# Dynamic convolution and gated MLP: head of the kernel reordered, and copies of weight rows issued later

## What is computed

```python
w = softmax(weight_gen, axis=-1)
conv[b, s, h, :] = sum(w[b, s, h, k] * x_pad[b, s + k, h, :] for k in range(7))
h = conv.reshape(16384, 192) @ w_in          # 192 x 2048
g = h * sigmoid(1.702 * h)
out = g @ w_out                              # 2048 x 192
```

## Time and profile before

| | before |
|---|---|
| median of 3 runs | 1126.83 us (1126.73 to 1127.22) |
| profiled execution, its own time | 1126.67 us |
| span of its trace | 1124.9 us |
| TensorE busy | 1111.5 us (99%) |
| VectorE / ScalarE / GpSimd busy | 802.1 / 622.0 / 12.8 us |
| bytes moved | 43.46 MB, mean 39 GB/s |

### The profile page before, as it was taken

The page is one execution under the profiler, slowest core; times in us unless marked ns, Lnnn a source line. Parts: engine busy times, 40 slices in busy tenths (PEclk is TensorE's granted clock), DMA queues, the critical chain, the costliest instruction groups (busy, mean ns, idle before and its releaser), DMA issues.

```text
span 1124.9 us, 21696 instructions
## 1 busy us (share of the span) xinstructions
PE 1111.5 (99%) x9748; PEld 915.3 (81%) x9748; DVE 802.1 (71%) x710; ACT 622.0 (55%) x661; POOL 12.8 (1%) x13
## 2 busy tenths in 40 slices
PE   6999999999999999999999999999999999999998
PEld 4888888888888888888888888888888888888886
DVE  7999988687685966859668496785858768587322
ACT  7767655464645555455464554645555555454543
POOL 2100000000000000000000000000000000000000
PEclk9999999999999999999999999999999999999999
DMA  8801010101001010010100101010010100100000
GB/s 274 238 15 54 15 54 1 39 29 40 29 2 39 29 40 29 1 57 12 40 29 18 51 1 40 29 40 29 1 40 29 40 29 1 40 29 1 29 1 29
DMA packets 9980, 43.46 MB, mean 39 GB/s; under 512 B 1120, under 2 KB 2400, under 8 KB 7584
## 3 DMA queue, kind: packets, MB, share of 16 engines
q1 hardware_dynamic: 8400, 40.51, 10.9%
q0 software_dynamic: 1488, 1.57, 0.9%
HBM read 24.77 MB, written 12.58 MB: 33 GB/s over the span
## 4 chain that ended last, share of the span: by engine, by line
PE 98%; DVE 1%; DMA 0%; issue 0%; ACTq 0%; DVEq 0%; SPq 0%; ACT 0%
PE hid L655 47%; PE acc_main L671 31%; PE acc_rest L671 21%; DMA gate<-in_x_first 0%; DVE hid L489 0%; DVE prod L483 0%; PE acc_main L622 0%; DVE hid L483 0%; DVE outs_main L511 0%; ACTq L73 0%; DVE outs_rest L552 0%; DVEq L73 0%; PE acc_rest L622 0%; SPq L199 0%; ACT outs_main L304 0%
## 5 line engine op out<-in xcount | busy, mean ns | idle before, releaser
L317 ACT ACTIVATE gate<-hid 128x1024 f32<-128x1024 f32 x256 | 263.1, 1028 | 480.0 <-PE hid L655 479.4
L568 DVE TENSOR_TENSOR gate_lo<-gate,gate_hi 128x1024 fp32r<-128x1024 f32 x256 | 312.9, 1222 | 260.6 <-ACT gate_hi L320 260.5
L655 PE MATMUL hid<-xt,w_hi 64*128 64x512 f32 x3072 | 431.5, 386 | 0.0
L655 PEld LDWEIGHTS hid<-xt,w_hi 64*128 64x128 f32 x3072 | 287.7, 184 | 61.6 <-ACT gate_hi L320 0.8
L671 PE MATMUL acc_main<-gate_hi,w 64*128 64x512 f32 x2048 | 315.8, 386 | 0.0
L320 ACT ACTIVATE gate_hi<-hid 128x1024 fp32r<-128x1024 f32 x256 | 260.7, 1018 | 0.0
L671 PEld LDWEIGHTS acc_main<-gate_hi,w 64*128 64x128 f32 x2048 | 191.9, 184 | 40.3
L655 PE MATMUL hid<-xt,w_lo 64*128 64x512 f32 x1536 | 215.8, 386 | 0.0
L671 PE MATMUL acc_rest<-gate_hi,w 64*128 64x512 f32 x1024 | 199.6, 386 | 0.0
L671 PE MATMUL acc_rest<-gate_lo,w 64*128 64x512 f32 x1024 | 199.6, 386 | 0.0
L671 PE MATMUL acc_main<-gate_lo,w 64*128 64x512 f32 x1024 | 199.6, 386 | 0.0
(11 more groups left out here) (57 smaller groups left out, 229.7 us busy)
## 6 DMA issues: line engine op xcount, KB each, us to landing
xwin<-in_x_runs SPq DMA_DIRECT2D x15, 1056.0 KB, 4.9
out<-outs_main SPq DMA_DIRECT2D x13, 512.0 KB, 2.6
out<-outs_rest SPq DMA_DIRECT2D x13, 256.0 KB, 2.9
taps<-in_tap_runs SPq DMA_DIRECT2D x1, 3136.0 KB, 10.4
taps<-in_w_rows SPq DMA_DIRECT2D x2, 1536.0 KB, 9.6
w_hi<-w_hi SPq DMA_DIRECT2D x2, 768.0 KB, 10.4
w_lo<-w_lo SPq DMA_DIRECT2D x2, 768.0 KB, 8.7
out<-outs_main SPq DMA_DIRECT2D x6, 256.0 KB, 2.0
```

The lines of the kernel that those rows point to most:

```text
L317: nc.scalar.activation(gate[:, v % 2, :, :], hid[:, v % 2, :, :], ACT.Gelu_apprx_sigmoid).then_inc(gate_ready, 1)
L568: nc.vector.tensor_tensor(gate_lo[:, v % SLOTS, :, :], gate[:, v % 2, :, :], gate_hi[:, v % SLOTS, :, :], ALU.subtract).then_inc(gate_lo_r ...
L655: last = nc.tensor.matmul(hid[:, v % 2, h, :], w[rows, k if j else slice_of(h, k), q, f], xt[rows, j % 2, part, k, :], start=(i == 0), sto ...
```

## The change

TensorE takes over part of the head's sum. It multiplies VectorE's product 0 (its first 512 columns) and GpSimd's three products by the identity and accumulates them in PSUM (`head_pile`); GpSimd's addition goes, and its third product is made in two halves. VectorE adds its products 1 and 2, then product 0's last 256 columns, then product 3, and the closing sums add this to the pile. The identity is loaded with `x_first`, as 128 more columns. The warm-up is 16 matmuls of 128 columns of zeros, which GpSimd sets first. All three rounded slices of piece 0 are written by ScalarE; unit 0 takes its terms slice by slice; its `gate_hi` is a copy of its gate, and unit 2 waits for the gate alone. `w1` is rounded in two halves, and GpSimd, not ScalarE, negates the later half, in two parts with a transfer each. The early remainder of `w2` moves from unit 2 to unit 1 on VectorE. On SP, the `w1_hi` copies move behind the wait for the late remainders, in front of the `w1_lo` copies.

```diff
-WARM_UP = 4
+WARM_UP = 16
...
-        head_prod = [prod[:, k, 0:N_FIRST] for k in range(2)]
-        shared_prod = [prod[:, 0, N_FIRST:N_CONV], prod[:, 1, N_FIRST:N_CONV], conv[:, 0:N_FIRST]]
+        first_flat = gate[:].rearrange("p b h n -> p (b h n)")[:, 0:FIRST_WIN * D + P]
+        ident = first_flat[:, FIRST_WIN * D:FIRST_WIN * D + P]
+        head_prod = [prod[:, 0, 0:N_FIRST], prod[:, 0, N_FIRST:N_CONV], prod[:, 1, 0:N_FIRST]]
+        head_sum = prod[:, 1, N_FIRST:N_CONV]
+        shared_prod = [conv[:, 0:N_FIRST], conv[:, N_FIRST:N_CONV], head_more[:]]
...
-            sp.dma_start(x_head, x_first).then_inc(x_loaded, 16)
+            sp.dma_start(first_flat, x_first).then_inc(x_loaded, 16)
...
-            sp.dma_start(ident[:], identity).then_inc(ident_loaded, 16)
...
-            sp.wait_ge(w1_hi_ready, 1)
+            sp.wait_ge(w1_lo_ready, 3)
+            sp.wait_ge(w1_late_ready, 2)
+            sp.wait_ge(w1_hi_ready, 2)
             sp.dma_start(w1_hi[LOWER, :, 1, :].bitcast(F32), w1_hi[UPPER, :, 0, :].bitcast(F32)).then_inc(w1_doubled, 16)
             sp.dma_start(w1_hi[UPPER, :, 1, :].bitcast(F32), w1_hi[LOWER, :, 0, :].bitcast(F32)).then_inc(w1_doubled, 16)
-            sp.wait_ge(w1_lo_ready, 3)
-            sp.wait_ge(w1_late_ready, 2)
...
-            nc.scalar.activation(w1_hi[:, :, 0, :], w1_raw, ACT.Copy).then_inc(w1_hi_ready, 1)
-
-            act.wait_ge(w1_hi_ready, 1)
-            nc.scalar.activation(w1_lo[:, :, 0, LATE], w1_hi[:, :, 0, LATE].bitcast(F32), ACT.Copy, scale=-1.0
-                                 ).then_inc(w1_negated, 1)
+            for cols in (EARLY, LATE):
+                nc.scalar.activation(w1_hi[:, :, 0, cols], w1_raw[:, :, cols], ACT.Copy).then_inc(w1_hi_ready, 1)
...
-            for k in (0, 2):
+            for k in range(SLICES):
                 act.wait_ge(head_turned_ready, k + 1)
-                nc.scalar.activation(xt[:, 0, 0, k, :], head_turned[k], ACT.Copy).then_inc(head_hi_act, 1)
+                nc.scalar.activation(xt[:, 0, 0, k, :], head_turned[k], ACT.Copy).then_inc(head_hi, 1)
...
+                    if n == 0:
+                        act.wait_ge(gate_ready, 1)
+                        nc.scalar.activation(gate_hi[:, 0, :, :], gate[:, 0, :, :], ACT.Copy).then_inc(gate_hi_ready, 1)
...
+                mul(0, head_prod[0])
+                mul(1, head_acc)
                 mul(2, head_prod[1])
+                mul(3, head_prod[2])
+                dve.wait_ge(head_op, 7)
+                add(head_acc, head_acc, head_prod[1])
+                dve.wait_ge(head_op, 9)
+                add(head_acc[:, N:N_FIRST], head_acc[:, N:N_FIRST], head_prod[0][:, N:N_FIRST])
                 dve.wait_ge(head_op, 10)
+                add(head_sum, head_acc, head_prod[2])
                 dve.wait_ge(head_op, 11)
+                dve.wait_ge(head_piled, 1)
...
-            dve.wait_ge(head_turned_ready, 2)
-            nc.vector.tensor_copy(xt[:, 0, 0, 1, :], head_turned[1]).then_inc(head_hi_dve, 1)
...
-                    if n == 2:
+                    if n == 1:
                         w2_remainder(2, SOON)
...
+            for i, first, last in ((0, 0, FIRST), (1, 0, FIRST), (2, 0, FIRST // 2), (2, FIRST // 2, FIRST)):
...
-            nc.gpsimd.tensor_tensor(shared_prod[2], shared_prod[1], shared_prod[2], ALU.add).then_inc(shared_op, 1)
-            pool.wait_ge(w1_negated, 1)
-            pool.dma_start(w1_raw[:, :, LATE], w1_lo[:, :, 0, LATE].bitcast(F32), accum_op=ALU.add).then_inc(w1_added, 16)
+            pool.wait_ge(w1_hi_ready, 2)
+            for i, part in enumerate(LATE_PARTS):
+                nc.gpsimd.tensor_scalar(w1_lo[:, :, 0, part], w1_hi[:, :, 0, part].bitcast(F32), -1.0, None,
+                                        ALU.mult).then_inc(w1_negated, 1)
+                pool.wait_ge(w1_negated, i + 1)
+                pool.dma_start(w1_raw[:, :, part], w1_lo[:, :, 0, part].bitcast(F32), accum_op=ALU.add
+                               ).then_inc(w1_added[i], 16)
...
+                for _ in range(WARM_UP):
+                    nc.tensor.matmul(head_turned[0][:, 0:P], zeros, zeros, start=True, stop=True)
                 pe.wait_ge(x_loaded, 16)
...
                 pe.wait_ge(head_op, 5)
+                pile(head_prod[0], FORE, start=True)
+                pe.wait_ge(shared_op, 1)
+                pile(shared_prod[0], FORE)
+                pile(shared_prod[0], AFT, start=True)
+                pe.wait_ge(shared_op, 2)
+                pile(shared_prod[1], FORE)
+                pile(shared_prod[1], AFT)
+                pe.wait_ge(shared_op, 3)
+                pile(shared_prod[2], slice(0, WAY))
+                pe.wait_ge(shared_op, 4)
+                pile(shared_prod[2], slice(WAY, N), stop=True)
+                pile(shared_prod[2], AFT, stop=True).then_inc(head_piled, 1)
...
-                wait(pe, gate_hi_ready, n - 1)
+                if n == 2:
+                    pe.wait_ge(gate_ready, 1)
+                else:
+                    wait(pe, gate_hi_ready, n - 1)
...
+                if n == 0:
+                    terms = [(w, 0, k) for k in range(SLICES) for w in (w1_hi, w1_lo)] + terms[2 * SLICES:]
```

More of the change, by code:

```diff
@@ L33 @@
 CROSS_HI_AT, CROSS_LO_AT = (7, 7, 5), (7, 7, 5)
-WARM_UP = 4
+WARM_UP = 16
 SHARED = 3
 def ffn_of_dynamic_conv(nc: bass.Bass, x_runs: bass.AP, tap_runs: bass.AP, x_first: bass.AP, tap_first: bass.AP,
-                        identity: bass.AP, w1_rows: bass.AP, w2_rows: bass.AP, out: bass.AP):
+                        w1_rows: bass.AP, w2_rows: bass.AP, out: bass.AP):
     CB = x_runs.shape[2]
@@ L172, in slice_of @@
             return (k + h) % SLICES
+        EARLY, LATE = slice(0, FH // 2), slice(FH // 2, FH)
+        LATE_PARTS = (slice(FH // 2, FH * 3 // 4), slice(FH * 3 // 4, FH))
         SOON = CH // 4
         LATE_CHUNKS = ((SOON, SOON + 2), (SOON + 2, CH // 2))
[L176 removed]
         MAIN, MAIN_LO = slice(0, P), slice(2 * P, 3 * P)
@@ L583, in _ @@
         def _(pool):
+            nc.gpsimd.memset(zeros, 0.0).then_inc(zeros_ready, 1)
             pool.wait_ge(x_loaded, 16)
             pool.wait_ge(head_shared, 1)
-            g = FIRST * H
-            norm = tap_norm[:, 0:g * SHARED].rearrange("p (g k) -> p g k", k=SHARED)
-            for i in range(SHARED):
-                k = ALONE + i
-                nc.gpsimd.tensor_tensor(shared_prod[i].rearrange("p (g c) -> p g c", c=GRP),
-                                        x_head[:, k:k + FIRST, :].rearrange("p t (h c) -> p (t h) c", c=GRP),
-                                        norm[:, :, i:i + 1].broadcast_to([P, g, GRP]), ALU.mult).then_inc(shared_op, 1)
-            pool.wait_ge(shared_op, SHARED)
-            nc.gpsimd.tensor_tensor(shared_prod[2], shared_prod[1], shared_prod[2], ALU.add).then_inc(shared_op, 1)
-            pool.wait_ge(w1_negated, 1)
-            pool.dma_start(w1_raw[:, :, LATE], w1_lo[:, :, 0, LATE].bitcast(F32), accum_op=ALU.add).then_inc(w1_added, 16)
+            norm = tap_norm[:, 0:FIRST * H * SHARED].rearrange("p (g k) -> p g k", k=SHARED)
+            for i, first, last in ((0, 0, FIRST), (1, 0, FIRST), (2, 0, FIRST // 2), (2, FIRST // 2, FIRST)):
+                k, of = ALONE + i, slice(first * H, last * H)
+                nc.gpsimd.tensor_tensor(shared_prod[i].rearrange("p (g c) -> p g c", c=GRP)[:, of],
+                                        x_head[:, k + first:k + last, :].rearrange("p t (h c) -> p (t h) c", c=GRP),
+                                        norm[:, of, i:i + 1].broadcast_to([P, (last - first) * H, GRP]), ALU.mult
+                                        ).then_inc(shared_op, 1)
+            pool.wait_ge(w1_hi_ready, 2)
[5 more added lines that the diff above has]
+                               ).then_inc(w1_added[i], 16)
             for i, (at, to) in enumerate(LATE_CHUNKS):
@@ L606, in turn_head, with pile @@
             def turn_head():
-                flat = x_head.rearrange("p t d -> p (t d)")
+                pe.wait_ge(zeros_ready, 1)
+                for _ in range(WARM_UP):
+                    nc.tensor.matmul(head_turned[0][:, 0:P], zeros, zeros, start=True, stop=True)
                 pe.wait_ge(x_loaded, 16)
+                FORE, AFT, WAY = slice(0, N), slice(N, N_FIRST), N_FIRST // 2
+                def pile(part, cols, start=False, stop=False):
+                    return nc.tensor.matmul(head_pile[:, cols], ident, part[:, cols], start=start, stop=stop)
                 pe.wait_ge(head_op, 5)
-                for i in range(WARM_UP):
-                    nc.tensor.matmul(hid[:, 0, 0, :], flat[:, i * P:(i + 1) * P], flat[:, N:2 * N], start=True, stop=True)
-                pe.wait_ge(ident_loaded, 16)
+                pile(head_prod[0], FORE, start=True)
[10 more added lines that the diff above has]
+                pile(shared_prod[2], AFT, stop=True).then_inc(head_piled, 1)
                 for k in range(SLICES):
@@ L621, in turn_head @@
```

(9 more changed lines are left out.)

57 lines of the change are left out of this document (23 added, 34 removed).

## The result

| | before | after |
|---|---|---|
| median | 1126.80 us (6 runs) | 1131.02 us (6 runs, 1130.82 to 1131.46) |
| profiled execution, its own time | 1126.67 us | 1131.27 us |
| span | 1124.9 us | 1129.5 us |

The ratio is 1.0036, with a 95% interval of 1.0027 to 1.0046: slower by 4.2 us. The prediction was 1132.0.

A forecast was written before the change was run, and what follows sets the result against it. TensorE, busy 99% of the span, was taken to bound the kernel. The median 1126.83 plus 5.1 us for the late window, already containing the head's 1.15 gain, gave 1131.9, stated as 1132.0; range 1129.5 to 1134.5.

The forecast's parts named there:

- The row copies: In SP's queue, the moved w1_hi copies delay piece 2's window to 64.2, making second product 14 5.1 us late.
- VectorE's 22.07 us in one piece: VectorE works without idle from piece 2's first product to unit 14's remainder; TensorE has 0.55 us of room there.
- the term 7.4 us: Delay of piece 2's window by two more w1_hi copies ahead in SP's queue: 1.57 MB at 213 GB/s.
- The head: The start of the kernel up to unit 4: the rearranged sum gives 1.1 to 1.2 us, ScalarE early by 1.15.
- the closing sums' 1.16: In the head, the closing sums start at 12.3 instead of 13.46, 1.16 us gained.
- 64 KB can cost only their share: The first load, grown from 960 to 1024 KB, takes nothing to 0.31 us more; 0.16 was taken.
- The wait of 0.3 before unit 4: In the head, TensorE was to wait about 0.3 us before unit 4, with ScalarE what is late next.
- A: Rival at SP's queue: the copies do not hold up piece 2's window, only the head counts, 1125.6; chance 0.10.
- B: Rival at SP's queue: the copies run at the rate of loads, 4.2 us, giving 1128.7; chance 0.09.
- C: Rival at second product 10: TensorE's clock falls in the new wait, 1132.0 to 1134.2; chance 0.15 for over 0.5 us.
- the 2.2 us of later waits: After the 4.0 us wait at second product 10, TensorE's shorter waits at units 11 and 14.
- D: Rival in the head: zeros do not raise the clock, the head loses 1.0 instead of winning 1.16, 1134.2; chance 0.06.

The follow-up runs named there:

- e2: The kernel before, with only both w1_hi copies moved behind the wait for the late remainders, in front of the w1_lo copies; 1132.65 us, ratio 1.0049.
- e5: The kernel before, with only the second w1_hi copy moved behind the wait for the late remainders; 1128.73 us, ratio 1.0017.
- e8: e3 with the identity loaded by a transfer of its own behind the first x; 1125.13 us, ratio 0.9986.
- e7: e3 with GpSimd's negations held back until VectorE has made the three early remainders of w1; 1125.68 us, ratio 0.9989.
- e1: The changed kernel with the two w1_hi copies issued early again, as soon as w1 is rounded; 1125.82 us, ratio 0.9989.
- e4: The changed kernel with the window of piece 2 issued ahead of the taps, the copies left in place; 1125.58 us, ratio 0.9989.
- e6: e3 without the 16 multiplications of zeros; 1127.44 us, ratio 1.0006 to the kernel before.
- e3: The changed kernel with all four copies of w1 rows issued behind the window of piece 2; 1125.84 us, ratio 0.9991.
- e10: The changed kernel itself measured and profiled once more, with nothing changed; 1131.18 us, ratio 1.0039.
- e9: e8 with e7's wait added, so the identity is loaded apart and the negations are held back; 1125.42 us, ratio 0.9988.

## Why the prediction was right, point by point

**The row copies: right, and the cost a little too high.** The way from SP's queue over the window, VectorE's 22.07 us in one piece and the 0.55 us of room to second product 14 held in all its steps: from 63.84 to the weight load of second product 14 at 85.97 it was 22.13, the 22.07 and the hand-over. What was mis-sized is the term 7.4 us. The window landed 5.85 later than before although it was issued 0.75 earlier, which makes the copies 6.6 us, 238 GB/s; by the same reckoning they cost 6.9 in e2 (landing at 65.16, with a first x 0.26 later), and e5's single one 3.1. Why they ran faster than the 213 GB/s of 16:22 is not shown. That stretch also held the end of piece 1's window, until about 17.6, but 18:20, behind it, gave 215 as well; after the change the four stretches of 2 us in 42:50 gave 221 to 233.

**The head: right in the steps, too good in the size.** It was put at 1.15 us and ScalarE showed 0.75 in the profiled execution. Of the closing sums' 1.16, 0.51 came; 0.60 is the first x, which landed at 6.7 instead of 6.1. That 64 KB can cost only their share was the weak step; the profiles with and without them differ by 0.3 on average, and single executions by more. Part of this was made good by luck: the first activation came 4.67 after the sums, not 4.93, so 0.24 were gained on ScalarE behind the sums where the prediction had nothing (0.14 - 0.15). The pile itself took what it should (7.83 to the sums at 12.95, 5.1 against 5.0), and it, not VectorE, set the sums, as said. In e8, where the first x came early, the head gave 1.6 at unit 4, with the stall of unit 1 absent too. The wait of 0.3 before unit 4 that was forecast is not in the changed kernel, since TensorE came later than ScalarE there.

**A wait not foreseen.** The negations were costed on GpSimd and on whoever waits for them, with a bound of 1.82 us (they took 2.14 and 2.66), but not on VectorE, which works beside them. The first of the two remainders took 1.67 us instead of 0.55. In the changed kernel that costs TensorE 0.34, and some 0.3 of it reaches unit 4 (28.53, where ScalarE would have let it load at 28.22). The sum did not suffer, because the window's landing hangs on ScalarE: SP issued the first copy 0.76 early, like gate_hi. In the kernels without the late window it is worth 0.3 by the rows (e7, e8).

**The two errors offset in part.** Cheaper copies took 0.8 us off and the later ScalarE put 0.4 on: 4.7 in the profiled execution instead of 5.1, and 4.2 by medians. That they have opposite signs is luck.

**The rivals.** A fell with e1, e2 and e4: the window could not overtake. B fell with the rate. C happened, and cost nothing. The stretch 68.5:72 after the wait of 3.2 us (instead of the 4.0 forecast), with the columns of the earlier trace rows:

```profile
68.50:72.00 3.50, 3.40 (x16) 2.71 (x18) 3.43 (x7) 2.68 (x4) 0.00 (x0) 0.51 0.00 0
```

The granted clock was 0.51, the lower level, and second product 10 took 3.7 us until the next first product instead of 2.3; the extra 1.4 and the 0.76 that TensorE still waited at unit 14 are together the 2.2 us of later waits that the prediction had left to it. In e5, with waits of 1.1 and 1.2 us, the clock stayed at 1.00; in e2, after 3.75 us, it stood at 1.00 in 70:71, with TensorE back at work, and then fell too (0.75, 0.50 and 0.50 in 71:74). The Trainium skill's "TensorE: Matmul & The Clock Gate" (HAM oscillation) has idle between bursts throttle the array; both profiles of the changed kernel agree. D is what e6 shows, and its price of 2.2 (the 1.16 not won and 1.0 lost) was 1.6 against e3.

## What to carry to other kernels

A transfer that nobody needs soon is not free to move later: ask what stands behind it in its queue, when that lands, and how much room its reader has. Here two copies whose rows are first read by unit 40's first product, at 185 us before and after (not near 193, as e3's expectation has it), cost 5.8 us, because a load needed at 58 us stood behind them; behind that load they cost nothing. And an engine that works without a pause turns one late load into a delay of equal length for everything in its order, so the room must be looked for at the end of its busy stretch, not at the first wait.

## What the runs showed that was not expected

- GpSimd's negation of 128x768 from SBUF held up those VectorE operations with two inputs from SBUF that started after it; what decided was which of the two began first. Second negation and pair of remainders, in the changed kernel and in e4 (timelines):

```profile
16.80 2.66 POOL L595 TENSOR_SCALAR w_lo<-w_hi 128x768 fp32r<-128x768 f32 x1
16.88 1.67 DVE L452 TENSOR_TENSOR w_lo<-taps,w_hi 128x384 fp32r<-128x384 f32 x1
18.48 0.95 DVE L452 TENSOR_TENSOR w_lo<-taps,w_hi 128x768 fp32r<-128x768 f32 x1
```

```profile
16.93 0.55 DVE L452 TENSOR_TENSOR w_lo<-taps,w_hi 128x384 fp32r<-128x384 f32 x1
16.98 2.66 POOL L595 TENSOR_SCALAR w_lo<-w_hi 128x768 fp32r<-128x768 f32 x1
17.39 1.75 DVE L452 TENSOR_TENSOR w_lo<-taps,w_hi 128x768 fp32r<-128x768 f32 x1
```

  Begun 0.08 behind the negation, the first remainder took 1.67 instead of 0.55, and unit 1 waited for it (likewise in e1, e3 and e10). Begun 0.05 or 0.14 ahead (e4, e8), it took its 0.55; the second remainder took 1.75 or 1.83 instead of 0.95, and nobody waited. It is not a fixed factor: beside the first negation (13.33, 2.14 us) the same operation, begun 0.62 behind, took 0.61, and in e8, begun 0.38 behind, 0.84. Begun 2.36 behind the second negation (e6), it took 0.55. If a held operation does its usual work once it is let go, that moment is, as an estimate, 0.68 us after the start of a negation of 2.14 us, 0.97 to 0.99 after one of 2.42 or 2.43 (e7, e9) and 1.20 after one of 2.66: always about 1.45 before the marked end. VectorE's products beside GpSimd's products, one input of VectorE's being in PSUM, keep their 0.95. One case is not explained: in e6 the first remainder took 0.90 with no negation beside it, while GpSimd issued a transfer (15.30, 1.47 us).

  The Trainium skill's "SBUF — State Buffer" (two separate sides) states such a lock for VectorE operations with two SBUF inputs against a GpSimd operation that reads SBUF, gives it to whichever starts first, and has the other wait for the whole instruction. That the first to start wins agrees with the changed kernel, e1, e3, e4, e8 and e10. The whole instruction, as the profile marks it, does not agree, though the profile's spans of GpSimd are rough.
- SP's third and fourth copy took 2.78 and 2.29 us to issue with two in flight ahead of them, against 0.6 before (2.81 and 2.31 in e2). The number ahead in the queue does not decide it: in e3 the same four copies, behind the taps and the window, took 0.73, 0.60, 0.62 and 0.65. The cause stays open. Here it cost nothing, since the next issue waited for the weights.
- Executions with the same load differ by up to 0.64 us in when the first x is there (VectorE's first product at 6.17 in e7 and 6.81 in e4), more than most of the head's edits are worth.
